# Where two stages meet: first feed-forward products placed between the last mixing products, and token work spread over more steps

## The reference

```python
X = np.fft.rfft(x, axis=1)
Yr = Xr @ w_r - Xi @ w_i + b_r
Yi = Xr @ w_i + Xi @ w_r + b_i
Y  = sign(Y) * maximum(abs(Y) - 0.01, 0)          # both parts
y  = np.fft.irfft(Y, n=3008, axis=1)
h  = y @ w_in;  g = maximum(h, 0) + alpha * minimum(h, 0);  z = g @ w_out      # layer 1
h  = z @ w_in2; g = where(h >= 1, h, where(h <= -1, 0, (h + 1)**2 / 4))        # layer 2
out = g @ w_out2
```

## Time and profile before

| | us |
|---|---|
| median of 3 timed runs | 1197.14 (1196.1 to 1198.14) |
| profiled execution, its own time | 1194.89 |
| its span, first to last instruction | 1193.1 |
| PE busy | 1173.4 (98%) |
| PEld busy | 1135.1 (95%) |
| DVE, ACT, POOL busy | 886.8, 850.2, 691.8 |

### The profile page before, as it was taken

The page is one execution under the profiler, slowest core; times in us unless marked ns, Lnnn a source line. Parts: engine busy times, 40 slices in busy tenths (PEclk is TensorE's granted clock), DMA queues, the critical chain, the costliest instruction groups (busy, mean ns, idle before and its releaser), DMA issues.

```text
span 1193.1 us, 21060 instructions
## 1 busy us (share of the span) xinstructions
PE 1173.4 (98%) x6948; PEld 1135.1 (95%) x6948; DVE 886.8 (74%) x1686; ACT 850.2 (71%) x1874; POOL 691.8 (58%) x724
## 2 busy tenths in 40 slices
PE   8999999999999999999999999999999999999997
PEld 3899889999999999999999999999999999999997
DVE  4777677777777777777778787778778787878765
ACT  2335557777777777777767788888878787878775
POOL 3006546666575766766556566665657575757553
PEclk9999999999999999999999999999999999999999
DMA  9777620211112101212005500101010101010001
GB/s 307 247 251 238 189 66 1 94 40 54 41 49 72 67 27 41 85 37 67 19 1 177 190 23 2 26 1 27 1 27 1 27 1 24 4 19 9 13 15 27
DMA packets 64125, 77.75 MB, mean 65 GB/s; under 512 B 31216, under 2 KB 43632, under 8 KB 64016
## 3 DMA queue, kind: packets, MB, share of 16 engines
q1 hardware_dynamic: 60532, 69.92, 19.0%
q10 hardware_dynamic: 3484, 6.48, 1.6%
HBM read 46.10 MB, written 30.28 MB: 64 GB/s over the span
## 4 chain that ended last, share of the span: by engine, by line
PE 93%; POOL 3%; ACT 1%; DVE 1%; issue 1%; DMA 1%; SPq 0%; POOLq 0%; DVEq 0%; ACTq 0%
PE bank L1153 80%; PE bank L1120 6%; PE bank L1139 2%; PE bank L1094 2%; PE bank L1130 2%; PE bank L1105 2%; POOL g_lo L515 2%; DMA x_sb<-x 1%; POOL prep_raw L541 0%; POOL xc_lo L490 0%; PE bank L1078 0%; ACT g_hi L762 0%; ACT prep_hi L785 0%; SPq L325 0%; DVE y_sum L856 0%
## 5 line engine op out<-in xcount | busy, mean ns | idle before, releaser
L515 POOL TENSOR_TENSOR g_lo<-g_sb,g_hi 128x376 fp32r<-128x376 f32 x510 | 505.1, 1001 | 374.2 <-ACT g_hi L762 373.7
L1153 PE MATMUL bank<-g_hi,w_out_hi 128*128 128x376 f32 x1024 | 345.1, 337 | 0.9 <-POOL g_lo L515 0.4
L1153 PE MATMUL bank<-g_lo,w_out_hi 128*128 128x376 f32 x1024 | 342.0, 334 | 0.0
L1153 PE MATMUL bank<-g_hi,w_out_lo 128*128 128x376 f32 x1024 | 341.8, 334 | 0.0
L1153 PE MATMUL bank<-xc_hi,w_in_hi 128*128 128x376 f32 x896 | 302.3, 337 | 0.6 <-DVE partial L921 0.2
L1153 PE MATMUL bank<-xc_hi,w_in_lo 128*128 128x376 f32 x896 | 300.4, 335 | 0.0
L1153 PE MATMUL bank<-xc_lo,w_in_hi 128*128 128x376 f32 x896 | 298.5, 333 | 0.0
L762 ACT ACTIVATE g_hi<-g_sb 128x376 fp32r<-128x376 f32 x512 | 261.0, 510 | 44.1 <-DVE g_sb L958 28.5
L1153 PEld LDWEIGHTS bank<-g_hi,w_out_hi 128*128 128x128 f32 x1024 | 192.3, 188 | 8.8 <-POOL g_lo L515 7.6
L1153 PEld LDWEIGHTS bank<-g_lo,w_out_hi 128*128 128x128 f32 x1024 | 192.4, 188 | 0.0
L1153 PEld LDWEIGHTS bank<-g_hi,w_out_lo 128*128 128x128 f32 x1024 | 192.3, 188 | 0.0
(11 more groups left out here) (82 smaller groups left out, 1534.3 us busy)
## 6 DMA issues: line engine op xcount, KB each, us to landing
gc<-group_consts SPq DMA_DIRECT2D x24, 256.0 KB, 4.3
zt<-slots_scratch SPq DMA_DIRECT2D x24, 256.0 KB, 4.2
inverse_scratch<-v_sb SPq DMA_DIRECT2D x24, 256.0 KB, 2.8
ut<-inverse_scratch SPq DMA_DIRECT2D x16, 384.0 KB, 4.8
slots_scratch<-a_sb ACTq DMA_DIRECT2D x15, 384.0 KB, 4.2
x_sb<-x SPq DMA_DIRECT2D x16, 256.0 KB, 4.0
prep_raw<-wpack SPq DMA_DIRECT2D x16, 256.0 KB, 2.6
out<-yt SPq DMA_DIRECT2D x120, 32.0 KB, 1.6
```

What stands on the lines that cost most here:

```text
L515: pool.tensor_tensor(g_lo[kind][:, :], g_sb[n % 3][:, :], g_hi[kind][:, :].bitcast(f32), ALU.subtract)\
L1153: done = pe.matmul(out_ap, w, g, start=first and n == 0, stop=last_one and n == 2, skip_group_check=unchecked)
```

## The change

It has three parts. On TensorE, the last token job moves from step 42 to step 44, and the seam gets a new order: P1 of group 0 before `mix(46)`, P6 before `inverse(45)`, P2 before `inverse(46)`, P5 ahead of P7, then `inverse(47)`, and P1 and P6 of group 1 ahead of P4 and P3 of group 0. On VectorE and ScalarE, the token operations of the first pair get steps of their own: at most one per step on VectorE. VectorE's copy of P1 (`take_p1`) is cut out of `make_u2`, and is done in step 47 for group 0 and after `make_c12(0)` for group 1. Last, the waits for operands are divided: each product of a pair's first group waits for its own operand (`low_part`), and the weight blocks are waited for one by one.

```diff
-TOKEN_STEPS = {36: 0, 38: 1, 40: 2, 42: 3}
+TOKEN_STEPS = {36: 0, 38: 1, 40: 2, 44: 3}
@@ GpSimd
-                if s == 44:
+                if s == 45:
                     token_lo(0, T3, r[2][:, :])
-                if s == 46:
-                    token_lo(0, T4, r[1][:, :])
+            token_lo(0, T4, r[1][:, :])
@@ ScalarE, steps: before, T1 40, B22 41, T2 42, B21 and T3 43, T4 45
+                if s == 40:
+                    turned_hi(0, 1, T1, r[1])
+                if s == 41:
+                    side_hi(0, 2, B22)
+                if s == 42:
+                    turned_hi(0, 2, T2, r[0])
+                if s == 44:
+                    turned_hi(0, 3, T3, r[2])
+                if s == 45:
+                    side_hi(0, 3, B21)
+                if s == 47:
                     turned_hi(0, 4, T4, r[1])
-            take_v(STEPS - 2)
@@ ScalarE, group 0, after first_part(0, C11)
                 if g == 0:
+                    take_v(STEPS - 2)
                     take_v(STEPS - 1)
@@ VectorE
+            def take_p1(g):
+                dve.wait_ge(p1_done, g + 1)
+                if g:
+                    dve.wait_ge(h_ready[C22], g)
+                else:
+                    dve.wait_ge(win_lo_ready, FP)
+                    dve.wait_ge(wout_lo_ready, FP)
+                dve.tensor_copy(partial[:, :], c11_bank[:, 0:N]).then_inc(p1_left, 1)
             for s in range(STEPS):
                 split_xt(s)
+                if s == STEPS - 1:
+                    take_p1(0)
                 if s:
                     threshold(s - 1)
@@ VectorE, steps: before, t1 39, t2 and B22 41, t3 42, B21 43, t4 44
+                if s == 41:
                     side_t2(0)
+                if s == 42:
                     side_lo(0, 2, B22)
+                if s == 43:
+                    side_t3(0)
+                if s == 45:
                     side_lo(0, 3, B21)
+                if s == 46:
                     side_t4(0)
@@ VectorE, groups
+                if 1 < g < ALL_GROUPS:
+                    take_p1(g)
                 if g < ALL_GROUPS:
                     make_u2(g)
...
                     make_c12(g)
+                    if g == 0:
+                        take_p1(1)
                     second_part(g, C21)
@@ TensorE
+            def low_part(q, which):
+                if q < TILE_PAIRS and which in (B11, B22, B21):
+                    pe.wait_ge(b_lo_ready, 3 * q + (B11, B22, B21).index(which) + 1)
+                else:
+                    pe.wait_ge(t_lo_ready, t_lo_count(q, which))
             def make_p1(g):
                 q, fp = divmod(g, FP)
                 if fp == 0:
-                    if q < TILE_PAIRS:
-                        pe.wait_ge(b_lo_ready, 3 * q + 3)
-                    pe.wait_ge(t_lo_ready, t_lo_count(q, T4))
-                if g == 0:
-                    pe.wait_ge(win_lo_ready, FP)
+                    low_part(q, B11)
+                if q == 0:
+                    pe.wait_ge(win_lo_ready, fp + 1)
@@ and low_part in make_p6 (T2), p2 (B21), p7 (T3), p5 (T1), p4 (T4), p3 (B22); in make_out
-                    pe.wait_ge(wout_lo_ready, FP)
+                if q == 0 and nth == 0:
+                    pe.wait_ge(wout_lo_ready, fp + 1)
@@ TensorE, steps
+                if s == STEPS - 1:
+                    make_p1(0)
                 if s:
                     mix(s - 1)
+                if s == STEPS - 1:
+                    side_free(0, 4)
+                    make_p6(0)
                 if s >= 2:
                     inverse(s - 2)
-            side_free(0, 4)
-            for g in range(ALL_GROUPS + 1):
+            mix(STEPS - 1)
+            make_p2(0)
+            inverse(STEPS - 2)
+            make_p5(0)
+            pe.wait_ge(y_ready, STEPS)
+            make_p7(0)
+            inverse(STEPS - 1)
+            make_p1(1)
+            make_p6(1)
+            make_p4(0)
+            make_p3(0)
+            for g in range(1, ALL_GROUPS + 1):
```

More of the change, by code:

```diff
@@ L710, in _ @@
                 weights_hi(s)
-                job = TOKEN_STEPS.get(s - 1)
-                if job == 0:
+                if s == 37:
                     side_copy(0, 0, r[0])
                     side_hi(0, 0, B11)
-                if job == 1:
+                if s == 39:
                     side_copy(0, 1, r[2])
-                if job == 2:
+                if s == 40:
+                    turned_hi(0, 1, T1, r[1])
+                if s == 41:
                     side_hi(0, 2, B22)
-                if job == 3:
-                    side_hi(0, 3, B21)
[L721 to L729, removed]
+                if s == 42:
[3 more added lines that the diff above has]
+                if s == 45:
+                    side_hi(0, 3, B21)
+                if s == 47:
                     turned_hi(0, 4, T4, r[1])
-            take_v(STEPS - 2)
             act.wait_ge(half_ready, 1)
@@ L1177, in make_p6 @@
             def make_p6(g):
+                if g % FP == 0:
+                    low_part(g // FP, T2)
                 q, at = divmod(g - 1, FP)
@@ L1185, in make_p2 @@
             def make_p2(g):
+                if g % FP == 0:
+                    low_part(g // FP, B21)
                 pe.wait_ge(p1_left, g + 1)
@@ L1189, in make_p7 @@
             def make_p7(g):
+                if g % FP == 0:
+                    low_part(g // FP, T3)
                 if g:
@@ L1194, in make_p5 @@
             def make_p5(g):
+                if g % FP == 0:
+                    low_part(g // FP, T1)
                 if g:
@@ L1199, in make_p4 @@
             def make_p4(g):
+                if g % FP == 0:
+                    low_part(g // FP, T4)
                 pe.wait_ge(u3_ready, g + 1)
@@ L1203, in make_p3 @@
             def make_p3(g):
+                if g % FP == 0:
+                    low_part(g // FP, B22)
                 pe.wait_ge(h_ready[C22], g + 1)
@@ L1245, in _ @@
                     tokens(0, TOKEN_STEPS[s])
-            side_free(0, 4)
-            for g in range(ALL_GROUPS + 1):
+            mix(STEPS - 1)
[10 more added lines that the diff above has]
+            for g in range(1, ALL_GROUPS + 1):
                 q, at = divmod(g, FP)
-                if g < ALL_GROUPS:
+                if 1 < g < ALL_GROUPS:
                     make_p1(g)
                     make_p6(g)
-                if g == 0:
-                    mix(STEPS - 1)
-                    inverse(STEPS - 2)
                 make_out(g - 1, 0)
@@ L1261, in _ @@
                     make_p2(g)
-                if g == 0:
-                    inverse(STEPS - 1)
-                if g < ALL_GROUPS:
                     make_p7(g)
```

## The result

| | before | changed |
|---|---|---|
| timed median, 12 executions each | 1197.14 us | 1193.89 us |
| profiled execution | 1194.89 | 1193.44 |
| span | 1193.1 | 1191.6 |

The ratio is 0.9971, with a 95% interval of 0.9962 to 0.998: 3.5 us faster, between 2.4 and 4.5. The forecast was 2.7 us and 1194.4. But the profiled executions differ by 1.45 us only, and that had to be explained too. One execution of the kernel before, in the measurement of experiments 1 to 4, took 1476.35 us at a mean granted clock of 0.752; no ratio here uses it.

What follows compares the result with a forecast made beforehand. TensorE was taken as the bound, full from 170 us on, with some 4.5 us idle in the last FFT steps and seam. 3.34 gained less 0.64 lost gives 2.7 us, from 1197.14 to 1194.4; range 1192.8 to 1196.6.

Steps and rivals of the forecast that it cites:

- Token job 3 without a wait, a new one at mix(42): TensorE, last FFT steps: losses of 2.60 and 1.10 us removed, a new 0.40 us wait on y_sum at mix(42).
- No further wait up to step 47: TensorE after mix(42): each later mix finds its y_sum ready, so 0 us more is lost through step 47.
- The margins of 0.02 to 0.2: Slack of y_sum before its mix: 0.17, 0.17 and 0.33 us, less the 0.15 from y_sum to TensorE.
- P1's wait on C11: Seam, TensorE: P1 of group 1 waits 0.89 us for g_ready of C11, starting at P + 1.94.
- P: Seam, TensorE: the start of P7 of group 0, predicted at E + 1.60 = 158.20 us.
- the sum: Link-by-link addition of times: 3.34 us gained up to E, 0.64 lost in the seam, 2.7 us net.
- P2 and the output products of C21: Seam, TensorE: P2 of group 1 starts at E + 7.45, C21's output products at E + 9.60 (166.20 us).
- E: TensorE: start of what follows mix(47), 159.94 us before the change, predicted at 156.60.
- C22's second part at 0.60: Seam, VectorE: this operation, starting at P + 4.25, takes 0.60 us rather than its 1072 ns median.
- The exclusion: Rival at C22's second part: VectorE with two SBUF inputs excludes GpSimd's SBUF reads; 0.46 us more, 1194.9, chance 0.08.
- The added waits at nothing: TensorE's list: some 102 more waits cost zero, upper bound 6.1 us; the rival that they cost had chance 0.08.
- The clock: TensorE's granted clock: 1.00 in all three stretches, so no gap was taken to cost speed behind it.

Runs made afterwards that it cites:

- experiments 1 to 4: Edits of the changed kernel: old seam order, 1194.31 us; old token steps, 1198.04; group 0's C22 output before C21's, 1192.44; first ut loads a pair earlier, 1193.29.
- experiment 7: Kernel before with VectorE's side_t3 moved ahead of threshold(41) in step 42: 1195.52 us, ratio 0.9987.
- experiment 2: Changed kernel with its new seam order, but token job 3 and the token operations back in the old steps: 1198.04 us, ratio 1.0004.

## Why the prediction was right, point by point

- *Token job 3 without a wait, a new one at mix(42)*: right. Job 3 has no idle time; mix(42) starts 0.76 after forward(43), 0.40 over the 0.36 of an unhindered one.
- *No further wait up to step 47*: right, in both profiles of the changed kernel and in the new steps with the old seam: TensorE is busy for 4.00 of the 4.00 us from 146 us on and for 10.00 of the 10.00 from 150 us on in all three. The margins of 0.02 to 0.2 held.
- *P1's wait on C11*: 0.89 predicted, start to start from P + 1.05 to P + 1.94. P7 started at 159.31 and P1 of group 1 at 161.40: 2.09, 0.15 later than predicted: u3 came 0.05 later than the sum had it, and P1 started 0.15 behind the end of the second part, not 0.05. Idle 0.88, by the duration column.
- *P2 and the output products of C21*: E + 7.45 and E + 9.60 predicted, E + 7.53 and E + 9.68 measured. VectorE's order of operations was the chain; each of its links came 0.1 later behind P7 than predicted.
- *C22's second part at 0.60*: right, 0.60 at 163.68; GpSimd's low part of C11 ran from 161.88 to 162.89. The exclusion that the Trainium skill states (SBUF — State Buffer, "SBUF: two separate sides") was not put to the test in this kernel's seam, since the two never met there; in the rest of the stage the median of that operation is 1071 ns, as it was 1072.
- *The added waits at nothing*: right; the feed-forward stage is unchanged to 0.01 us of busy time in 920, and from the second output products to the end it takes 1024.2 us in both.

Three things were missed, and none of them in a step of the sum. **The clock.** The prediction says that no gap costs speed behind it, since the clock was 1.00 in all stretches. That was true of one execution. Behind the same 2.43 us gap two of five profiles have a half clock, for 3.4 and 6.8 us, so removing the gap is worth 0.9 us more on average than its length. **The load of `ut`.** Before token job 0 TensorE is idle for 0.08 to 2.25 us in every kernel but those with the early load, and this shifts whole profiles against each other. **The start.** Profiles differ by up to 2.3 us already at forward(26).

With the clock, 2.66 + 0.9 = 3.6 us stands against the measured 3.5 (2.4 to 4.5) and 4.2 (2.8 to 5.6). The load and the start add nothing to the difference of the two kernels: from forward(36) to job 0 it takes 3.85 us on average over six profiles with the old steps and 3.76 over five with the new ones, and forward(36) starts at 121.8 and 121.9 on average.

The three together explain most of why the kernel before has a median 2.25 above its first profiled execution. Its four profiles average 1.46 above that first one: 0.44 by the start up to forward(36), 0.60 up to job 0, and 0.40 by the one fall of the clock among them. That low mean clocks go with the old steps is shown, by 31 of 64 executions against 0 of 40; that it makes up 0.9 us, and so just the difference between 2.66 and 3.5, rests on five profiles and agrees with the mean clocks.

## What to carry to other kernels

Time a rearrangement by two or three intervals inside the trace, from a point that nothing has touched yet to the point where the engine is full again: here they were right to 0.1 us, while the spans of two profiled executions misled by 1.2. An operation put ahead on the bottleneck engine can make the whole result later, if it waits for something that others behind it would have produced meanwhile; ask of every reordering whose input comes last, and put that producer first (P4 ahead of P1 and C22's output ahead of C21's gave 1.0 us each, against the 0.7 that the new seam had cost). Take the clock of several profiles, and the mean clock of the timed executions, before a gap of some 2 us is called free.

## What the runs showed of the hardware that was not expected

After the same 2.43 us without a matmul, TensorE's granted clock fell from 2.4 to 1.2 GHz in two profiles (0.50 and 0.57 in the stretches behind) and not in three, with the same instructions on both sides of the gap. Behind the 1.18 us gap of experiment 7, and behind the idle time before token job 0 (1.32 us in the changed kernel, 2.25 in experiment 2), the next products kept their full pace.

The new steps do not keep the clock up everywhere. In nine of the 13 profiles, the changed kernel's first among them, it falls to 0.50 for 3.4 us near the start of the kernel, beginning between 25.7 and 33.9 us, where TensorE waits for loads of x. The stretch from 10 to 50 us, first in the kernel before, where it does not fall, then in the changed kernel:

```profile
10.00:50.00 40.00, 35.55 (x162) 21.34 (x160) 20.65 (x46) 13.52 (x32) 0.00 (x0) 1.00 0.84 285
10.00:50.00 40.00, 36.63 (x161) 21.85 (x160) 20.61 (x45) 13.66 (x32) 0.00 (x0) 0.96 0.83 284
```

The last wait before these falls was 1.32 to 2.96 us long (2.15 in the changed kernel's first profile). The four profiles without a fall have waits of 2.16 to 2.53 us there, so the length of one wait does not tell by itself. The nine reach forward(26) at 97.9 us on average, and so do the four: there the fall cost nothing that can be seen.
